# A decayed-attention and two-MLP kernel: blocks of up to 512 tokens, decays by scans, and a shorter first plan

## The chip, the cores and the metric

The kernel runs on one core of a Trainium2 chip. The metric is the device time of one execution in microseconds, as the median of several runs. A profile of one execution stands beside it, with the work of TensorE (PE), VectorE (DVE), ScalarE (ACT), GpSimd (POOL) and the DMA queue that SyncE (SP) issues.

## What is computed

Linear attention with a decay per key channel, then two MLPs, all in float32:

```python
# q, k, v, alpha: (4, 8, 768, 48); alpha in 0.8 to 1.0
for t in range(S):
    state = alpha[:, :, t, :, None] * state + np.einsum('bhd,bhe->bhde', k[:, :, t], v[:, :, t])
    y[:, :, t] = np.einsum('bhd,bhde->bhe', q[:, :, t], state)
x = y.transpose(0, 2, 1, 3).reshape(3072, 384)
h = x @ w_in                                   # 384 x 2048
x = (np.maximum(h, 0) + a * np.minimum(h, 0)) @ w_out
h = x @ w2_in
x = np.where(h >= 1, h, np.where(h <= -1, 0, (h + 1) ** 2 / 4)) @ w2_out
```

## The kernel before

**Units.** The sequence is cut into chunks of 128 tokens; a unit is one chunk of one batch with its eight heads, 24 units in all, six to a batch. Two heads lie in one tile, one on partitions 0 to 47 and one on 64 to 111, so four pairs. For a unit the running product of alpha over the chunk (prod) and its inverse (inv) are formed; q is multiplied by prod and k by inv; the scores are masked and multiplied by v; and a state of 48x48 per head is carried from chunk to chunk.

**Stages of a unit.** "product" and "product_end": seven doubling passes over prod (L218, after a copy L212), 112x256 each, on DVE (unit 2 on POOL). "inverse": the last column kept (p_last, L512), a reciprocal of every fourth column (L515), three passes that fill the columns between (L518), k times inv (L522), all DVE; POOL multiplies q by prod (L343). "scores": PE transposes k (L658) and forms the scores (L664), ACT copies k to token-major order (k_tok, L405), DVE masks (L528). "mix": PE forms the state sums (L674) and the outputs (L684 with the state, L688 with v), ACT copies the outputs (L411), DVE updates the state (L551, L555). "turn": PE transposes the outputs (L702), ACT rounds them into x_hi (L418), DVE subtracts for x_lo (L561). A batch's first unit has no L684; its last one has no L674, but has its key transposes.

**The MLPs.** A block is 384 tokens, three units. There are eight blocks in each layer, and a step is one tile of 128 hidden channels of a block, 16 steps to a block. Every float32 product is made of three float32r products, high part times low, high times high, low times high (L723 to L725). In a step PE does the hidden product of the step two ahead (nine matmuls of 384 columns into one of two h_ps banks) and then the output product of this step (nine more, into y_ps). Between them ACT takes a relu (L433), DVE combines (L568 in the first layer, L576 and L579 in the second), ACT rounds into g_hi (L439), and POOL subtracts into g_lo (L350). g32, g_hi and g_lo have four slots each. x_hi and x_lo have two, so a block's units are made while the block before is multiplied.

**The order.** Each engine works in the order of its program; semaphores tie the engines. In step f of a block every engine first does the unit stages that BLOCK_PLAN gives to the step, then its part of the activation of step f + 2:

```python
BLOCK_STAGES = {0: "product", 1: "product_end", 2: "inverse", 3: "scores", 4: "mix", 5: "turn"}
BLOCK_PLAN = [[(BLOCK_STAGES[f - 4 * j], j) for j in range(UPB) if f - 4 * j in BLOCK_STAGES] for f in range(FT)]
```

So unit j of the next block starts at step 4j, and its stages take six steps in a row. The three units of block 0 are made ahead of all products by FIRST_PLAN, with idle matmuls of PE between its stages (FILL, WARM).

**Weights.** Each weight tile (768 columns, input and output part) is loaded raw into w_raw (RAW = 3 slots), rounded into w_hi by ACT (L400), and its low parts are formed by POOL (L335, input part) and DVE (L503, output part). In block 0 one tile is split in each step; the second layer's tiles are split in the first layer's last block. The blocks but the first and last of a layer are loops of two block bodies. Outputs go to y_all and from there to memory after their block.

Of the kernel before, what the change touches and what calls it, by code (L numbers as in the profile page):

```python
# [10 lines left out]
P = 128  # L33
# [8 lines left out]
TOK = 384  # L42
UPB = TOK // CHUNK
BLOCKS = BATCH * SEQ // TOK
# [3 lines left out]
G_RING = 4  # L48
RAW = 3
AHEAD = 2  # L50
LEVELS = CHUNK.bit_length() - 1
SECOND = BLOCKS * FT

BLOCK_STAGES = {0: "product", 1: "product_end", 2: "inverse", 3: "scores", 4: "mix", 5: "turn"}
BLOCK_PLAN = [[(BLOCK_STAGES[f - 4 * j], j) for j in range(UPB) if f - 4 * j in BLOCK_STAGES] for f in range(FT)]

FIRST_PLAN = [("product", 0), ("product_end", 0), ("inverse", 0), ("product", 2), ("product_end", 2), ("product", 1),  # L60
              ("scores", 0), ("product_end", 1), ("inverse", 1), ("mix", 0), ("inverse", 2), ("scores", 1), ("turn", 0),
              ("mix", 1), ("scores", 2), ("turn", 1), ("mix", 2), ("turn", 2)]
BY_POOL = 2
SPARE = 2


WARM = 27
FILL = {("scores", 0): 3, ("mix", 0): 10, ("turn", 0): 6, ("turn", 1): 0, ("mix", 2): 2, ("turn", 2): 5}


def build_program(nc, qka, v, w, alpha, out):
    with ExitStack() as ctx:
# [7 lines left out]

        w_hi = sb("w_hi", [P, FT, WCOLS], F32R)
        w_lo = sb("w_lo", [P, FT, WCOLS], F32R)
        w_raw = sb("w_raw", [P, RAW, WCOLS])

        x_hi = sb("x_hi", [P, 2, KT, TOK], F32R)
        x_lo = sb("x_lo", [P, 2, KT, TOK], F32R)

        y_all = sb("y_all", [P, BLOCKS, KT, TOK])
        g32 = sb("g32", [P, G_RING, TOK])
# [14 lines left out]
        ident = sb("ident", [P, P])  # L104

        h_ps = [ctx.enter_context(nc.psum_tensor(f"h_ps{i}", [P, 512], F32)) for i in range(2)]
# [6 lines left out]
        unit_loaded = [sem(f"unit_loaded{i}") for i in range(3)]  # L113
        raw_loaded = [sem(f"raw_loaded{i}") for i in range(RAW)]
        slopes_loaded = sem("slopes_loaded")
        alpha_loaded = sem("alpha_loaded")
        slopes_set = sem("slopes_set")
        stored = sem("stored")
        pads_set = [sem(f"pads_set{i}") for i in range(3)]
        state_cleared = sem("state_cleared")  # L120
        ident_set = sem("ident_set")
        causal_set = sem("causal_set")
        w_hi_done = sem("w_hi_done")
        w_lo_in_done = sem("w_lo_in_done")
        w_lo_out_done = sem("w_lo_out_done")
        product_done = sem("product_done")
        first_done = sem("first_done")
        pool_product_done = sem("pool_product_done")
        pool_first_done = sem("pool_first_done")
        last_kept = sem("last_kept")  # L130
        inv_done = sem("inv_done")
# [13 lines left out]
        x_lo_done = sem("x_lo_done")  # L145
        h_done = sem("h_done")
# [8 lines left out]


        spare = y_all[:, BLOCKS - 2:].rearrange("p n m t -> p (n m t)")

        def qka_of(u):
            if u == SPARE:  # L160
                return spare[:, 0:3 * PAIRS * CHUNK].rearrange("p (x h t) -> p x h t", x=3, h=PAIRS)
            return qka_sb[:, u % 2]

        def v_of(u):
            return spare[:, 3 * PAIRS * CHUNK:3 * PAIRS * CHUNK + D_MODEL] if u == SPARE else v_sb[:, u % 2]

        def prod_of(u):

            if u != BY_POOL:
                return prod  # L170
            return y_all[:, BLOCKS - 3].rearrange("p m t -> p (m t)")[:, 0:PAIRS * CHUNK].rearrange(
                "p (h t) -> p h t", h=PAIRS)
# [9 lines left out]
        def out_bank(u):  # L182

            return y_ps[2] if u in (1, 2) else t_ps

        def product_of(u, levels):

            if u == BY_POOL:
                return pool_product_done, levels
            return product_done, LEVELS * (u - (u > BY_POOL)) + levels  # L190

        def product_stages(eng, turn, u, levels):

            done, first = (pool_product_done, pool_first_done) if u == BY_POOL else (product_done, first_done)
            out = prod_of(u)[0:ROWS]
            if levels[0] == 0:
                if u == 0:
                    eng.wait_ge(alpha_loaded, 32)
                else:
                    eng.wait_ge(loaded_of(u), at(turn, 48 * UPB, loads_of(u)))  # L200
                if u != BY_POOL:

                    ge(eng, q_scaled, turn, UPT, u)
                    ge(eng, k_scaled, turn, UPT, u)
                    ge(eng, last_kept, turn, UPT, u)
            for level in levels:
                half = 1 << level
                x, y = (t.rearrange("p h t -> p (h t)").rearrange("p (n two s) -> p n two s", two=2, s=half)
                        for t in (out if level else qka_of(u)[0:ROWS, 2], out))
                count = product_of(u, level)[1]  # L210
                if level == 0:
                    eng.tensor_copy(y[:, :, 0], x[:, :, 0]).then_inc(first, 1)  # L212
                else:
                    eng.wait_ge(done, at(turn, LEVELS * UPT, count))
                if level == 1:
                    eng.wait_ge(first, at(turn, UPT, count // LEVELS + 1))
# [589 lines left out]
```

## Time and profile before

| | us |
|---|---|
| median of 3 runs | 1038.96 |
| lowest, highest | 1036.35, 1043.89 |
| span of the profiled execution | 1046.5 |
| PE busy in it | 980.5 |
| DVE busy | 525.3 |
| POOL busy | 361.9 |
| ACT busy | 318.0 |

The span goes from the first to the last instruction of the profiled execution, which is an execution of its own and not one of the three. In rows of instructions the first number is the start in us from the span's start, the second the duration; a bracket gives the idle time of the engine before it and what ended it. PE rows overlap, since matmuls are pipelined: the time from start to start is what one costs. PE's float32 matmuls appear as two records each, those of float32r as one.

### The profile page before, as it was taken

The page shows a single profiled execution, that of the slowest core. Times are in us where ns is not written, and L with a number is a line of the kernel's source. Part 1 is how long each engine was busy: PE and PEld are TensorE (multiplying, and loading weights), DVE is VectorE, ACT ScalarE, POOL GpSimd, SP SyncE. Part 2 cuts the span into 40 slices and gives each one's busy share as a digit, 9 for nine tenths or more (in the row PEclk, how much of TensorE's full clock was granted, in tenths as well). Part 3 has the DMA queues.
Part 4 walks back from the last instruction along what each step waited for, and adds up shares of the span by engine and source line. Part 5 has one row for each costly group of instructions (what it writes and reads, how often), then busy time and mean ns, then how long its engine had stood idle before and what let it go on. Part 6 is the DMA issues. An engine that isn't in the chain of part 4 may idle for free.

```text
span 1046.5 us, 17070 instructions
## 1 busy us (share of the span) xinstructions
PE 980.5 (94%) x5970; PEld 961.8 (92%) x5970; DVE 525.3 (50%) x908; ACT 318.0 (30%) x673; POOL 361.9 (35%) x354
## 2 busy tenths in 40 slices
PE   7977799999999999989998999999999999999998
PEld 7877799898889898889897999999999999999998
DVE  8577666556457466367377244333333333333332
ACT  1332232222222222222232355333333333333232
POOL 4233332222232232223123287434343434333333
PEclk9888899998899898899899999999999999999999
DMA  5413211201111201302102032000000000000000
GB/s 136 106 61 91 61 31 31 53 9 32 41 22 34 56 2 31 58 4 54 37 1 76 1 107 90 2 23 1 24 1 23 0 23 0 23 0 23 0 24 23
DMA packets 14923, 37.02 MB, mean 35 GB/s; under 512 B 2224, under 2 KB 8368, under 8 KB 14864
## 3 DMA queue, kind: packets, MB, share of 16 engines
q1 hardware_dynamic: 14864, 36.19, 14.3%
q8 instruction: 42, 0.69, 0.3%
q14 instruction: 17, 0.14, 0.0%
HBM read 31.47 MB, written 4.72 MB: 35 GB/s over the span
## 4 chain that ended last, share of the span: by engine, by line
PE 76%; DVE 16%; issue 5%; DMA 1%; ACT 1%; POOL 1%; DVEq 0%; SPq 0%; POOLq 0%
PE h_ps L723 11%; PE h_ps L725 11%; PE h_ps L724 11%; PE y_ps L723 10%; PE y_ps L724 10%; PE y_ps L725 10%; DVE prod L218 4%; DVE inv L518 3%; PE a_ps L688 3%; PE a_ps L664 3%; DVE qka_sb L522 2%; DVE inv L515 2%; PE a_ps L684 2%; PE t_ps L658 1%; PE t_ps L674 1%
## 5 line engine op out<-in xcount | busy, mean ns | idle before, releaser
L350 POOL TENSOR_TENSOR g_lo<-g,g_hi 128x384 fp32r<-128x384 f32 x256 | 261.5, 1021 | 652.6 <-ACT g_hi L439 550.6
L433 ACT ACTIVATE g<-h_ps 128x384 f32<-128x384 f32 x256 | 126.0, 492 | 499.9 <-PE h_ps L725 499.9
L723 PE MATMUL h_ps<-x_lo,w_hi 128*128 128x384 f32 x768 | 269.6, 351 | 2.6 <-issue 2.6
L724 PE MATMUL h_ps<-x_hi,w_hi 128*128 128x384 f32 x768 | 262.9, 342 | 0.0
L725 PE MATMUL h_ps<-x_hi,w_lo 128*128 128x384 f32 x768 | 262.9, 342 | 0.0
L723 PE MATMUL y_ps<-g_lo,w_hi 128*128 128x384 f32 x768 | 259.2, 337 | 1.1 <-POOL g_lo L350 1.1
L724 PE MATMUL y_ps<-g_hi,w_hi 128*128 128x384 f32 x768 | 258.3, 336 | 0.0
L725 PE MATMUL y_ps<-g_hi,w_lo 128*128 128x384 f32 x768 | 257.7, 336 | 0.0
L576 DVE SCALAR_TENSOR_TENSOR g<-g 128x384 f32<-128x384 f32 x128 | 71.4, 558 | 244.8 <-ACT g L433 244.8
L723 PEld LDWEIGHTS h_ps<-x_lo,w_hi 128*128 128x128 f32 x768 | 148.4, 193 | 7.2 <-issue 5.8
L724 PEld LDWEIGHTS h_ps<-x_hi,w_hi 128*128 128x128 f32 x768 | 148.9, 194 | 0.0
L725 PEld LDWEIGHTS h_ps<-x_hi,w_lo 128*128 128x128 f32 x768 | 148.8, 194 | 0.0
L723 PEld LDWEIGHTS y_ps<-g_lo,w_hi 128*128 128x128 f32 x768 | 146.4, 191 | 1.9 <-POOL g_lo L350 0.9
L724 PEld LDWEIGHTS y_ps<-g_hi,w_hi 128*128 128x128 f32 x768 | 146.0, 190 | 0.0
L725 PEld LDWEIGHTS y_ps<-g_hi,w_lo 128*128 128x128 f32 x768 | 145.5, 189 | 0.0
L568 DVE SCALAR_TENSOR_TENSOR g<-g,slopes,h_ps 128x384 f32<-128x384 f32 x128 | 78.2, 611 | 126.0 <-ACT g L433 125.5
L439 ACT ACTIVATE g_hi<-g 128x384 fp32r<-128x384 f32 x256 | 132.8, 519 | 4.7 <-DVE g L568 3.9
L218 DVE TENSOR_TENSOR prod<-prod 112x256 f32<-112x256 f32 x138 | 85.7, 621 | 4.0
L579 DVE TENSOR_TENSOR g<-h_ps,g 128x384 f32<-128x384 f32 x128 | 71.3, 557 | 4.4
L658 PE MATMUL t_ps<-ident,qka_sb 112*128 112x112 f32 x88 | 16.0, 314 | 51.5 <-DVE qka_sb L522 51.5
L658 PEld LDWEIGHTS t_ps<-ident,qka_sb 112*128 112x128 f32 x88 | 10.4, 163 | 58.3 <-DVE qka_sb L522 53.1
L688 PE MATMUL a_ps<-v_sb,att 128*128 128x48 f32 x352 | 48.7, 266 | 0.7 <-DVE att L528 0.7
(83 smaller groups left out, 708.1 us busy)
## 6 DMA issues: line engine op xcount, KB each, us to landing
qka_sb<-qka SPq DMA_DIRECT2D x44, 288.0 KB, 4.7
w_raw<-w SPq DMA_DIRECT2D x32, 384.0 KB, 3.0
y<-y_all SPq DMA_DIRECT2D x24, 192.0 KB, 1.9
v_sb<-v SPq DMA_DIRECT2D x23, 192.0 KB, 4.8
y_all<-qka SPq DMA_DIRECT2D x2, 288.0 KB, 8.7
qka_sb<-qka SPq DMA_DIRECT2D x2, 192.0 KB, 3.5
qka_sb<-qka SPq DMA_DIRECT2D x2, 96.0 KB, 2.5
y_all<-v SPq DMA_DIRECT2D x1, 192.0 KB, 9.3
```

What stands on the lines that cost most here:

```text
L218: eng.tensor_tensor(y[:, :, 1], x[:, :, 1], left, ALU.mult).then_inc(done, 1)
L350: nc.gpsimd.tensor_tensor(g_lo[:, r], g32[:, r], g_hi[:, r].bitcast(F32), ALU.subtract).then_inc(g_lo_done, 1)
L433: nc.scalar.activation(g32[:, s % G_RING], h_ps[s % 2][:, 0:TOK], ACT.Relu, scale=-1.0 if s < SECOND else 0.5, bias=0.0 if s < SECOND else ...
L439: nc.scalar.activation(g_hi[:, s % G_RING], g32[:, s % G_RING], ACT.Copy).then_inc(g_hi_done, 1)
L568: nc.vector.scalar_tensor_tensor(out=g32[:, r], in0=g32[:, r], scalar=slopes[:, f:f + 1], in1=h_ps[s % 2][:, 0:TOK], op0=ALU.mult, op1=ALU ...
L576: nc.vector.scalar_tensor_tensor(out=g32[:, r], in0=g32[:, r], scalar=1.0, in1=g32[:, r], op0=ALU.min, op1=ALU.mult).then_inc(half_done, 1)
L579: nc.vector.tensor_tensor(g32[:, r], h, g32[:, r], ALU.max).then_inc(g_done, 1)
L658: last = nc.tensor.transpose(turn_bank(u)[:, h * P:h * P + ROWS], qka[0:ROWS, 1, h], ident[0:ROWS, 0:ROWS])
L688: last = nc.tensor.matmul(scores_bank(u, 0)[:, c], att[:, e, h], v_of(u)[:, c], start=fresh, stop=fresh or e == 1)
L723: nc.tensor.matmul(out_, wh, lo, start=start, stop=False)
L724: nc.tensor.matmul(out_, wh, hi, start=False, stop=False)
L725: last = nc.tensor.matmul(out_, wl, hi, start=False, stop=stop)
```

## The change

- Block sizes in units are (2, 3, 3, 4, 4, 4, 4) in the first layer and six of 4 in the second: 13 blocks and 208 steps instead of 16 and 256. A matmul of the products has 128 x size columns, 512 at most.
- Each unit's stages are planned back from its turn: decay 5 steps ahead, scores 3, mix 1. The last unit of a block turns at step 13 of the block before, the others 4 steps apart. Within a step the order is turn, scores, mix, decay.
- prod and inv come from scans: per unit four forward and four backward over 128 columns and a reciprocal of the last column of each pair. p_last is copied by POOL. No unit's product runs on POOL.
- The state sums go to the second scores bank instead of the turn bank. A batch's last unit has neither key transposes nor k_tok.
- FIRST_PLAN has two units; WARM and FILL are smaller. ACT splits weight tiles in between, ahead of copies of the plan; POOL makes both low parts of the first four tiles.
- g32 has two slots, g_hi and g_lo three. Raw weights of the first layer lie in eleven slots of y_all that is not yet written, those of the second layer in four slots where qka was.
- Loops are unrolled. The output array is (3, 128, 3072), with 512-byte pieces on the chip's side for each unit.
- SP loads unit u (from 2 on) when the outputs of unit u - 2 are done, instead of after its x_lo.

```diff
-TOK = 384
-G_RING = 4
-RAW = 3
+FIRST = (2, 3, 3, 4, 4, 4, 4)
+SECOND = (4, 4, 4, 4, 4, 4)
+SIZES = FIRST + SECOND
+TOK = CHUNK * max(SIZES)
+G32_RING, G_RING = 2, 3
+RAW_FIRST, RAW_SECOND = 11, 4
+EARLY = 4
-BLOCK_STAGES = {0: "product", 1: "product_end", 2: "inverse", 3: "scores", 4: "mix", 5: "turn"}
+for _n in range(1, N1):
+    for _j in range(SIZES[_n]):
+        _u, _turn = STARTS[_n] + _j, FT * (_n - 1) + 13 - 4 * (SIZES[_n] - 1 - _j)
+        for _stage, _lag in (("decay", 5), ("scores", 3), ("mix", 1), ("turn", 0)):
+            PLAN.setdefault(_turn - _lag, []).append((_stage, _u))
+ORDER = ("turn", "scores", "mix", "decay")
+FIRST_PLAN = [("decay", 0), ("decay", 1), ("scores", 0), ("scores", 1), ("mix", 0), ("turn", 0), ("mix", 1), ("turn", 1)]
+WARM = 20
+FILL = {("scores", 0): 3, ("scores", 1): 1, ("mix", 0): 4, ("mix", 1): 2, ("turn", 1): 3}
...
+            def decay(u):
+                al = qka_of(u)[0:ROWS, 2]
...
+                for h in range(PAIRS):
+                    nc.vector.tensor_tensor_scan(prod[0:ROWS, h], al[:, h], zeros[0:ROWS], 1.0,
+                                                 ALU.mult, ALU.add).then_inc(prod_done, 1)
+                dve.wait_ge(prod_done, PAIRS * (u + 1))
+                ge(dve, k_scaled, u)
+                nc.vector.reciprocal(inv[0:ROWS, :, CHUNK - 1], prod[0:ROWS, :, CHUNK - 1]).then_inc(inv_begun, 1)
+                dve.wait_ge(inv_begun, u + 1)
+                for h in range(PAIRS):
+                    nc.vector.tensor_tensor_scan(inv[0:ROWS, h, CHUNK - 2::-1], al[:, h, CHUNK - 1:0:-1],
+                                                 zeros[0:ROWS, 0:CHUNK - 1], inv[0:ROWS, h, CHUNK - 1:CHUNK],
+                                                 ALU.mult, ALU.add).then_inc(inv_done, 1)
...
                 nc.vector.tensor_tensor(k, k, inv[0:ROWS], ALU.mult).then_inc(k_scaled, 1)
...
+            splits = {("decay", 0): [0], ("decay", 1): [1, 2, 3]}
...
+                for i in splits.get(task, []):
+                    split_in(i)
+                    split_out(i)
...
+            splits = {("decay", 1): [0, 1], ("scores", 0): [2], ("scores", 1): [3], ("turn", 0): [4], ("turn", 1): [5]}
...
+            load_unit(0)
+            load_unit(1)
             sp.dma_start(slopes[:], alpha).then_inc(slopes_loaded, 16)
+            for i in range(6):
+                load_weights(i)
+            load_unit(2)
```

Of the two `splits`, the first is POOL's, after scale_q of the unit, and the second ACT's, after its own part of the stage.

## Rows read from the trace of the kernel before

**Rows 1.** The page: engines' busy time, and the granted clock in 40 slices.
```profile
PE 980.5 (94%) x5970; PEld 961.8 (92%) x5970; DVE 525.3 (50%) x908; ACT 318.0 (30%) x673; POOL 361.9 (35%) x354
...
PEclk9888899998899898899899999999999999999999
```

**Rows 2.** The view by stretches: start, first layer, second layer, tail.
```profile
core 0: us, PE busy (x) PEld busy (x) DVE busy (x) ACT busy (x) POOL busy (x), PEclk, DMA share, GB/s
...
42.90:646.10 603.20, 548.49 (x3423) 532.18 (x3422) 346.83 (x585) 177.78 (x367) 194.62 (x180) 0.93 0.20 46
646.10:1043.40 397.30, 396.70 (x2287) 396.06 (x2286) 146.72 (x264) 131.76 (x293) 151.98 (x151) 1.00 0.03 11
1043.40:1046.50 3.10, 0.00 (x0) 0.00 (x0) 0.04 (x1) 0.49 (x1) 0.00 (x0) 0.85 0.53 190
```

**Rows 3.** The waits of PE: total us, times, longest us.
```profile
PE t_ps L658 <- DVE qka_sb L522: 51.5, 21, 6.3
...
PE h_ps L723 <- issue: 2.6, 2, 1.5
```

**Rows 4.** Timeline of PE, one unit's stages at full clock.
```profile
170.37 0.60 PE L658 MATMUL t_ps<-ident,qka_sb 112*128 112x112 f32 x4 [1.22 <-DVE qka_sb L522]
170.90 1.16 PE L664 MATMUL a_ps<-qka_sb 48*128 48x128 f32 x16
172.00 0.44 PE L723 MATMUL h_ps<-x_lo,w_hi 128*128 128x384 f32 x1
...
175.23 0.93 PE L674 MATMUL t_ps<-v_sb,k_tok 128*112 128x96 f32 x8
176.00 0.39 PE L684 MATMUL a_ps<-state,qka_sb 112*128 112x96 f32 x2
...
178.62 0.42 PE L723 MATMUL h_ps<-x_lo,w_hi 128*128 128x384 f32 x1
...
181.83 0.49 PE L702 MATMUL t_ps<-ident,o_tok 128*128 128x128 f32 x3
182.08 0.42 PE L723 MATMUL h_ps<-x_lo,w_hi 128*128 128x384 f32 x1
```

**Rows 5.** Timeline of PE, the same stage behind a longer wait.
```profile
270.34 0.68 PE L658 MATMUL t_ps<-ident,qka_sb 112*128 112x112 f32 x4 [2.38 <-DVE qka_sb L522]
270.95 2.08 PE L664 MATMUL a_ps<-qka_sb 48*128 48x128 f32 x16
272.96 0.69 PE L723 MATMUL h_ps<-x_lo,w_hi 128*128 128x384 f32 x1
```

**Rows 6.** Groups by line and shape: busy us, mean ns, idle before.
```profile
L350 POOL TENSOR_TENSOR g_lo<-g,g_hi 128x384 fp32r<-128x384 f32 x256 | 261.5, 1021 | 652.6 <-ACT g_hi L439 550.6 <-issue 91.0 <-DVE g L568 10.9
...
L439 ACT ACTIVATE g_hi<-g 128x384 fp32r<-128x384 f32 x256 | 132.8, 519 | 4.7 <-DVE g L568 3.9 <-DVE g L579 0.8
...
L218 DVE TENSOR_TENSOR prod<-prod 112x256 f32<-112x256 f32 x138 | 85.7, 621 | 4.0
...
L568 DVE SCALAR_TENSOR_TENSOR g<-g,slopes,h_ps 128x384 f32<-128x384 f32 x128 | 78.2, 611 | 126.0 <-ACT g L433 125.5
...
L335 POOL TENSOR_TENSOR w_lo<-w_raw,w_hi 128x384 fp32r<-128x384 f32 x32 | 39.3, 1229 | 10.1 <-ACT w_hi L400 10.0
...
L518 DVE TENSOR_TENSOR inv<-inv,qka_sb 112x128 f32<-112x128 f32 x69 | 38.5, 557 | 2.4
...
L503 DVE TENSOR_TENSOR w_lo<-w_raw,w_hi 128x384 fp32r<-128x384 f32 x32 | 33.5, 1049 | 9.3 <-ACT w_hi L400 9.1
...
L522 DVE TENSOR_TENSOR qka_sb<-qka_sb,inv 112x512 f32<-112x512 f32 x23 | 22.3, 971 | 0.8
...
L515 DVE RECIPROCAL inv<-prod 112x128 f32<-112x128 f32 x23 | 21.8, 946 | 0.0
...
L218 DVE TENSOR_TENSOR prod<-qka_sb 112x256 f32<-112x256 f32 x23 | 10.4, 452 | 0.0
```

**Rows 7.** Timeline of DVE in the start: unit 1's decay begins, the last x_lo.
```profile
11.72 0.30 DVE L212 COPY prod<-qka_sb 112x256 f32<-112x256 f32 x1 [0.77 <-DMA v_sb<-v]
...
42.22 0.56 DVE L561 TENSOR_TENSOR x_lo<-y_ps,x_hi 128x384 fp32r<-128x384 f32 x1 [0.58 <-ACT x_hi L418]
```

More of the change, by code:

```diff
@@ L180, in turn_bank @@
             return y_ps[2] if u == 1 else t_ps
[L182 to L216, printed above, removed]
-                left = x[:, :, 0, half - 1:half].to_broadcast(x[:, :, 1].shape)
-                eng.tensor_tensor(y[:, :, 1], x[:, :, 1], left, ALU.mult).then_inc(done, 1)
@@ L359, in attention @@
-            def attention(turn, plan, first_unit):
-                for stage, j in plan:
-                    u = first_unit + j
-                    if stage == "product" and u == BY_POOL:
-                        product_stages(pool, turn, u, range(0, LEVELS))
-                    if stage == "inverse":
-                        scale_q(turn, u)
-            pool.wait_ge(pads_set[SPARE], 2)
-            attention(None, FIRST_PLAN, 0)
-            for i in range(RAW):
-                split_w(i)
@@ L373, in body @@
+            splits = {("decay", 0): [0], ("decay", 1): [1, 2, 3]}
+            for task in FIRST_PLAN:
+                if task[0] == "decay":
+                    scale_q(task[1])
+                for i in splits.get(task, []):
+                    split_in(i)
+                    split_out(i)
+            for n in range(BLOCKS):
                 for f in range(FT):
                     s = FT * n + f
-                    if n == 0 and f == 0:
-                        hidden_lo(turn, 0)
-                    if n == 0 and f + RAW < FT:
-                        split_w(f + RAW)
@@ L390, in _ @@
-            run(pool, body)
+                    if s == 0:
+                        hidden_lo(0)
+                    for stage, u in plan_of(s):
+                        if stage == "decay":
+                            scale_q(u)
+                    if s + 1 < STEPS:
+                        hidden_lo(s + 1)
+                    if n == 0 and f + EARLY < FT:
+                        split_in(f + EARLY)
+                    if N1 - 1 <= n < BLOCKS - 1 and 5 <= f < 5 + KT:
+                        input_lo(n + 1, f - 5)
@@ L452, in attention @@
[L452 to L464 removed]
+                    act.wait_ge(hidden_used, FT * (n + 1))
@@ L465, in _ @@
+            for stage, u in FIRST_PLAN:
+                if stage == "scores":
+                    copy_k(u)
+                if stage == "mix":
+                    copy_outputs(u)
+                if stage == "turn":
+                    turn_hi(u)
+                for i in splits.get((stage, u), []):
                     split_w(i)
             for s in range(AHEAD):
-                relu_of(None, s)
-            def body(turn, n):
+                relu_of(s)
+            for n in range(BLOCKS):
@@ L492, in _ @@
-            run(act, body)
-            copy_y(None, 2 * BLOCKS - 1, 0)
-            copy_y(None, 2 * BLOCKS - 1, 2)
+                        copy_y(n - 1, 0)
+                        copy_y(n - 1, 2)
+                    for stage, u in plan_of(s):
+                        if stage == "scores":
+                            copy_k(u)
+                        if stage == "mix":
+                            copy_outputs(u)
+                        if stage == "turn":
+                            turn_hi(u)
@@ L628, in body @@
+            for n in range(BLOCKS):
                 for f in range(FT):
@@ L642, in _ @@
-            run(dve, body)
-            copy_y(None, 2 * BLOCKS - 1, 1)
+                        copy_y(n - 1, 1)
+                    for stage, u in plan_of(s):
+                        if stage == "turn":
+                            turn_lo(u)
+                        if stage == "scores":
+                            mask(u)
+                        if stage == "mix":
+                            update_state(u)
+                        if stage == "decay":
+                            decay(u)
@@ L804 @@
     y = r.results[0]["y"]
[L805 removed]
+    return np.ascontiguousarray(y.reshape(D_MODEL, BATCH * SEQ).T)
```

664 lines of the change are left out of this document (321 added, 343 removed).

## The prediction

> **What bounds the kernel now.** I read the page first: PE (TensorE) is busy 94% of the span, and its granted clock dips from 1.0 to 0.8 or 0.9 in many slices of the first half and in none of the second [rows 1]. So TensorE sets the time, and the question is which of its microseconds are work. The view by stretches splits the span at three places of the trace: the first hidden product (42.9 us), the first matmul after the first layer's last output product (646.1 us) and the last matmul (1043.4 us) [rows 2]. The reader is to see that the two layers have the same matmuls (128 steps of 18) and that one takes 603.2 us, the other 397.3.
>
> The second layer gives the price of pure work: 397.3 us for 2,286 matmuls (2,304 less the 18 of the two steps issued ahead) is 173.8 ns for 384 columns, while the clock stays at 1.0, 2.4 GHz [rows 2]. 384 columns at 2.4 GHz are 160 ns, so 13.8 ns come on top of each matmul. The first layer's stretch holds 2,322 such matmuls, 403.6 us. The other 199.6 us are attention and loss.
>
> The attention work of one unit (128 tokens of one batch, all heads) is read off a unit at full clock, from start to start [rows 4]: key transposes 0.53 us, scores 1.10, state sums 0.77, outputs 2.62 (176.00 to 178.62), output transposes 0.25. Each return to the products costs 0.09 more, three times. That is 5.5 us. For a unit that opens a batch (no product with the state) it is 0.9 less, for one that closes it 0.8 less. The 21 units 3 to 23: 21 x 5.5 - 3 x 0.9 - 4 x 0.8 = 109.6 us.
>
> So 90 us of the first layer are lost. The waits of PE name 51.5 us of it: 21 waits, one per unit, of the key transposes for the scaled keys that DVE writes at L522, 6.3 us at most [rows 3]. Most of the rest is clock: behind a wait of 1.2 us the scores took 1.16 us, behind one of 2.4 us 2.08 us, and the first hidden matmul 0.69 instead of 0.44 [rows 4, 5]. TensorE had stood still before, and the records run at the lower level, 1.2 GHz. In the second layer, with no wait, nothing of that appears.
>
> Why is DVE late? A unit's decay work runs over three steps: seven products at L218 (the first 452 ns, the others 621), the reciprocal 946, three of L518 at 557, L522 971 [rows 6], with two short copies some 8.5 us in an engine that works in order. Between them it also stands behind the activations of the steps, which wait for hidden products that TensorE has yet to make. The scores come one step (3.13 us) after the last part.
>
> **The change, part by part.**
>
> *Decay by scans.* Seven doubling passes, the p_last copy and three inverse passes per unit leave DVE; 4 + 4 scans of 112x128, a reciprocal of 4 columns and the same L522 come. The trace has no scan. From below it is bounded by half of the first product (256 columns, 452 ns), 0.23 us; from above by the slowest row per column, the reciprocal of 128 columns, 0.95 [rows 6]. I take 0.45, between, and on the side of L518 (128 columns, 0.56 mean), because a scan divides nothing. Decay is then 8 x 0.45 + 0.16 (an estimate for the reciprocal of 4 columns, 946 less what 124 columns cost at 6 to 7 ns) + 0.97 = 4.7 us (2.9 to 8.7) in one piece. The Trainium skill, "DVE: opcode table, instruction layouts, handler registers and perf-mode slots", section "Datapath and trigger behaviour", says that this scan runs at half throughput. The trace of before has none to compare; by the page, 128 columns would take about what 256 take in a product, an estimate of 0.45.
>
> *Stages spaced apart.* Decay stands two steps ahead of the scores, and the scores two ahead of the mix. With four steps between units the decay of unit u+1 falls into the step of mix(u). Take T as this step's start on PE: outputs end at T+3.4, DVE's state update (four short ops, 1.5) at T+4.9, decay at T+9.6. PE reaches the scores two steps later: the mix 3.4 + two steps of products + the 0.3 of the turn. For 512-token blocks (step 4.1, below) that is T+11.9; for 384 (3.13) T+10.0; for 256 (2.2) T+8.1. So the wait is gone in the wide blocks, just gone at 384, and 1.5 us remain at the two units prepared that way in block 0. The activation queued on DVE behind the decay is needed a step later still: in a 384 block g is done at about T+10.2, g_lo 1.5 later (519 + 1,021 ns [rows 6]) at T+11.8, and the output product that needs it starts at T+13.2 (10.0 + 1.6 of scores + 1.6). Thin, no term. If this cover goes, every microsecond of decay more is a microsecond per unit. I leave 5 us of loss for block 0 and a cold start of the products. Gain 90 - 5 = 85.
>
> *Blocks of 512 with a ramp.* 13 blocks instead of 16: 208 steps, 3,744 matmuls instead of 4,608, the same columns. Whether the 13.8 ns is fixed per matmul or grows with the columns no row shows. Fixed (my choice: columns at 2.4 GHz should stream, something is paid at each change of weights): 512 takes 227 ns, the gain is 864 x 13.8 ns = 11.9 us. In proportion: 232 ns, gain nothing. Cost of the other engines at 512: ACT's copy 0.52 us to about 0.65 and the relu alike, DVE's combine 0.61 to 0.78, GpSimd's g_lo 1.02 to 1.36 [rows 6]; ACT has two of them in a step of 4.1, the others one. At 256, block 0 also splits weights: DVE 0.45 + 1.05 and GpSimd 0.7 + 1.23 in a 2.2 us step [rows 6], both near full, but TensorE has 16 us of attention in that block as cover. The Trainium skill, "TensorE: Matmul & The Clock Gate", section "Wait — 56ns, not 53.3ns?", has N/2.4 + 2.5 ns for a stream of matmuls: 162.5 at 384, where this trace has 173.8, so for this fp32r stream with a weight load each the measurement decides. By the page the 864 matmuls would be worth 2.2 us.
>
> *One unit moves from the start into the blocks, batch-closing units skip the key transposes.* 22 units instead of 21: +5.5. Closing units lose 4 x 0.53. Together +3.4.
>
> *The start.* Now unit 1's decay begins at 11.72, after a DMA had held it 0.77 us, and the third unit's x_lo at 42.22 releases the products at 42.92 [rows 7]. With two units: k of unit 0 scaled near 9, that of unit 1 near 14. But new queues form: ACT has splits 0 and 1 ahead of copy_k(0), and GpSimd has both halves of split 0 (2 x 1.23) ahead of scale_q(1), all behind the first weight's DMA, which is issued behind ten unit transfers and should land at 11 to 12. So scale_q(1) ends near 16, scores of unit 1 near 18.5 at the low clock, mix 0 at 22, o_tok and turn 24, mix 1 at 28, turn and x_lo of unit 1 near 31. First products at 31 (26 to 37) instead of 42.9: gain 11.9.
>
> *Weights staged in y space, RAW 3 to 11 and 4; unrolled; no third pad or POOL product.* The weights were in time already: PE waits for none of them [rows 3]. Nothing, hidden behind products. The loops leave no wait row on PE beyond a few "issue" microseconds [rows 3]; nothing, up to 3 us gain.
>
> *Tail.* The last copy and DMA are a third larger: 3.1 us [rows 2] to about 3.7, +0.6.
>
> Sum: 1046.5 - 85 - 11.9 + 3.4 - 11.9 + 0.6 = 941.7 us of span. The profiled span lies 7.5 us over the median of the runs (1038.96). The losses by waits and clock, which may differ from run to run, are nearly gone after, so I carry over only a little of that: **940 us**.
>
> **Rivals.**
> *A. The start stays long or block 0 binds.* For it: the new order on ACT and GpSimd above, and DVE near full in block 0. Against: two units instead of three. The start keeps its 42.9 and block 0 loses 5 more: 940 + 11.9 + 5 = 957 us.
> *B. Scans at the reciprocal's 0.95 us.* Decay 8.7: waits of 1.7 us at the 12 units prepared in 512 steps, 3.6 at 7 in 384, 5.5 at 3 in 256, 62 us, and some 15 of lower clock as now: 1017 us. Against: no division in a scan.
> *C. The 13.8 ns do not exist at 512 columns.* 2,880 wide matmuls x 13.8 = 40 us less: 900 us. The page's gap formula points this way, but the row at 384 speaks against it. The opposite, growth in proportion, is 952 us and inside the range.
> *D. Slower than before: the shorter rings.* g32 has two slots instead of four, so relu of step s+2 waits for g_lo of step s. The chain from h(s) to g_lo(s) is 0.65 + 0.78 + 0.65 + 1.36 = 3.4 us, and 8.2 us (two steps) are there. It decides from 8.2 on; the 105 us that lead back to 1046 need 0.5 us more in each of 208 steps, a chain of 9.2 us; at 9.3 it is 1,056 us. The decay in front of the activation reaches it once per unit, not per step.
>
> **Numbers.** Forecast case 0.70, A 0.18, B 0.05, C 0.04, D 0.02, the change not doing what it says (waits as now) 0.01. The range 922 to 966 holds the forecast with starts 26 to 37, a matmul price up to the proportional one and a decay up to 6 us, and reaches over A. Measurement of this kernel tells about 1% from no change. Faster by over 1%: 0.96 (all but D and part of B), within 1% 0.02, slower 0.02.
>
> **What would show it.** Key transposes without wait of over 1 us outside block 0; scores at 1.1 us throughout and the clock at 1.0 from about 35 us on; 512-column matmuls 227 ns apart; scan rows of 0.3 to 0.6 us; first hidden product at 26 to 37 us; the second layer 1,728 matmuls in about 391 us. Wrong if PE waits for g_lo or for a weight, if the scans take near 1 us, or if the clock dips with no wait in front of it.

## The result

The changed kernel takes 979.26 us (median of 4 runs, 975.71 to 981.99); the kernel before, run beside it, 1041.17. The ratio is 0.9414, 95% interval 0.9373 to 0.9455. The forecast was 940 us (922 to 966): the direction was right, about three fifths of the gain came, and the time lies outside the range. The span of the profiled execution is 980.3 us; the working of the prediction ended at 941.7.

| us | predicted | measured |
|---|---|---|
| start, to the first hidden product | 31 | 36.4 |
| products, 3,744 matmuls | 789 | 788.2 |
| attention of 22 units at full clock | 113 | 113 (taken as such) |
| waits and low clock between the products | 5 | 38.8 |
| tail | 3.7 | 3.9 |
| span | 941.7 | 980.3 |

The 788.2 us of products have two parts. The second layer's stretch below is 388.6 us, for 1,710 matmuls of 512 columns. The first layer's is priced from start to start of one matmul in the trace: 120 ns for 256 columns, 173.3 for 384, 226.7 for 512. It holds 288, 576 and 1,170 of them (18 of the last are the second layer's first two steps, issued ahead), 399.6 us. The 38.8 us are what is left of the first layer's 551.4 us (587.8 less 36.4) after these 399.6 and the 113 of attention.

The page of the changed kernel, engines' busy time and granted clock in 40 slices; it answers to [rows 1].

```profile
PE 946.6 (97%) x5050; PEld 815.9 (83%) x5050; DVE 448.1 (46%) x732; ACT 302.8 (31%) x561; POOL 354.8 (36%) x322
...
PEclk8777999999999999999999999999999999999999
```

The dips of the first half are gone, but for the first four slices. The view by stretches (start; block 0; the rest of the first layer; the second layer) shows the same, and answers to [rows 2].

```profile
core 0: us, PE busy (x) PEld busy (x) DVE busy (x) ACT busy (x) POOL busy (x), PEclk, DMA share, GB/s
0.00:36.40 36.40, 29.68 (x169) 28.31 (x169) 15.86 (x35) 8.83 (x13) 14.43 (x24) 0.72 0.69 196
36.40:113.20 76.80, 64.59 (x472) 61.66 (x472) 47.52 (x81) 24.57 (x55) 29.92 (x34) 0.84 0.27 62
113.20:587.80 474.60, 464.25 (x2704) 405.28 (x2703) 248.59 (x420) 147.57 (x277) 165.92 (x152) 1.00 0.20 42
587.80:976.40 388.60, 388.07 (x1711) 320.67 (x1709) 136.07 (x198) 121.26 (x218) 144.57 (x113) 1.00 0.04 11
```

Block 0 takes 76.8 us. Its products are 37.7 (288 matmuls of 256 columns, and 18 of 384 that belong to the first two steps of block 1) and its three units 16.5, so 22.6 of the 38.8 us are lost there: PE stands still for 12.2 of them, and the rest goes with a mean clock of 0.84. Blocks 1 to 5 have a stretch of their own:

```profile
113.20:522.50 409.30, 398.95 (x2415) 351.22 (x2414) 221.44 (x388) 116.53 (x225) 123.20 (x119) 1.00 0.19 37
```

With 296.6 us of products and 19 units at 5.5, the other 16.2 us are lost there, at full clock. PE stands still for 10.4 of them, in small waits; for the other 5.8 no view names a cause, and they may be units that cost somewhat more than 5.5 us. Block 6, with no unit in it, loses nothing (65.3 us for 288 matmuls).

The waits of PE in the changed kernel, total us, times, longest; they answer to [rows 3].

```profile
PE t_ps L607 <- DVE x_lo L518: 12.7, 12, 3.0
PE y_ps L670 <- POOL g_lo L303: 8.8, 10, 1.7
PE y_ps L607 <- POOL qka_sb L294: 4.7, 1, 4.7
PE t_ps L607 <- DVE qka_sb L480: 1.9, 2, 1.4
```

The 51.5 us of waiting for scaled keys have become 1.9. In their place stand two waits that were absent or small before (1.1 us for g_lo, none for x_lo): the key transposes for x_lo of the unit before (they write the bank t_ps from which DVE still has to form it), and the output products for g_lo. The third line of the four is one wait in the start.

The timelines of DVE and of POOL in the changed kernel, in the first step of block 5, which holds a mix and a decay.

```profile
440.51 0.74 DVE L511 TENSOR_TENSOR state<-state,p_last 48x192 f32<-48x192 f32 x2
441.28 1.37 DVE L467 TENSOR_TENSOR_SCAN prod<-qka_sb,zeros 112x128 f32<-112x128 f32 x4
442.69 0.18 DVE L471 RECIPROCAL inv<-prod 112x4 f32<-112x4 f32 x1
442.90 3.90 DVE L474 TENSOR_TENSOR_SCAN inv<-qka_sb,inv,zeros 112x127 f32<-112x127 f32 x4
446.84 0.69 DVE L480 TENSOR_TENSOR qka_sb<-qka_sb,inv 112x512 f32<-112x512 f32 x1
447.56 0.75 DVE L524 SCALAR_TENSOR_TENSOR g<-g,slopes,h_ps 128x512 f32<-128x512 f32 x1
448.23 0.55 DVE L518 TENSOR_TENSOR x_lo<-t_ps,x_hi 128x384 fp32r<-128x384 f32 x1
```

```profile
442.73 1.29 POOL L294 TENSOR_TENSOR qka_sb<-qka_sb,prod 112x512 f32<-112x512 f32 x1 [6.02 <-DVE prod L467]
443.96 0.20 POOL L297 COPY p_last<-prod 112x4 f32<-112x4 f32 x1
444.10 1.30 POOL L303 TENSOR_TENSOR g_lo<-g,g_hi 128x512 fp32r<-128x512 f32 x1
```

Two things are to be seen. POOL stood 6.02 us in front of scale_q (L294) until the forward scans had run, and g_lo of the next step was queued behind it. And four forward scans take 1.37 us, four reverse ones 3.90: beside the reverse ones POOL is at work from their start at 442.90 to 445.40, 2.5 us. In the start, with POOL quiet, four reverse scans took 1.60:

```profile
10.54 1.60 DVE L474 TENSOR_TENSOR_SCAN inv<-qka_sb,inv,zeros 112x127 f32<-112x127 f32 x4
```

The activation (L524) and x_lo (L518) follow only after the decay.

### The profile page after: what moved, and what is told of

It is laid out like the page before. It is cut to its first block, busy times and chain, and to the rows that moved or that the text cites. A ratio compares the mean times of both kernels' runs of the same rounds, so it can differ in the third digit from the quotient of the medians.

```text
span 980.3 us, 13041 instructions
## 1 busy us (share of the span) xinstructions
PE 946.6 (97%) x5050; PEld 815.9 (83%) x5050; DVE 448.1 (46%) x732; ACT 302.8 (31%) x561; POOL 354.8 (36%) x322
## 4 chain that ended last, share of the span: by engine, by line
issue 43%; PE 32%; POOL 20%; DVE 3%; DMA 1%; SPq 0%; ACT 0%; POOLq 0%; DVEq 0%; ACTq 0%
POOL g_lo L303 16%; PE h_ps L670 4%; PE y_ps L670 4%; PE y_ps L672 4%; PE y_ps L671 4%; PE h_ps L672 4%; PE h_ps L671 4%; PE a_ps L640 2%; POOL x_lo L310 2%; POOL w_lo L283 2%; PE a_ps L616 1%; PE a_ps L636 1%; PE a_ps L628 1%; DVE prod L467 1%; DVE inv L474 1%
## 5 line engine op out<-in xcount | busy, mean ns | idle before, releaser
L303 POOL TENSOR_TENSOR g_lo<-g,g_hi 128x512 fp32r<-128x512 f32 (+2 forms) x208 | 251.7, 1210 | 507.5 <-ACT g_hi L391 503.9
L384 ACT ACTIVATE g<-h_ps 128x512 f32<-128x512 f32 (+2 forms) x208 | 117.6, 565 | 493.9 <-PE h_ps L672 475.4
L670 PE MATMUL y_ps<-g_lo,w_hi 128*128 128x512 f32 (+2 forms) x624 | 234.4, 376 | 8.9 <-POOL g_lo L303 8.8
L670 PE MATMUL h_ps<-x_lo,w_hi 128*128 128x512 f32 (+2 forms) x624 | 240.9, 386 | 0.1
L672 PE MATMUL h_ps<-x_hi,w_lo 128*128 128x512 f32 (+2 forms) x624 | 234.2, 375 | 0.0
L671 PE MATMUL h_ps<-x_hi,w_hi 128*128 128x512 f32 (+2 forms) x624 | 233.9, 375 | 0.0
L672 PE MATMUL y_ps<-g_hi,w_lo 128*128 128x512 f32 (+2 forms) x624 | 233.3, 374 | 0.0
L671 PE MATMUL y_ps<-g_hi,w_hi 128*128 128x512 f32 (+2 forms) x624 | 233.3, 374 | 0.0
L524 DVE SCALAR_TENSOR_TENSOR g<-g,slopes,h_ps 128x512 f32<-128x512 f32 (+2 forms) x112 | 74.8, 669 | 142.9 <-ACT g L384 142.3
L391 ACT ACTIVATE g_hi<-g 128x512 fp32r<-128x512 f32 (+2 forms) x208 | 123.2, 592 | 31.3 <-DVE g L524 29.0
L474 DVE TENSOR_TENSOR_SCAN inv<-qka_sb,inv,zeros 112x127 f32<-112x127 f32 x96 | 81.2, 903 | 0.9
L294 POOL TENSOR_TENSOR qka_sb<-qka_sb,prod 112x512 f32<-112x512 f32 x24 | 30.8, 1284 | 103.9 <-DVE prod L467 101.0
```

The lines of the kernel that those rows point to most:

```text
L294: nc.gpsimd.tensor_tensor(q, q, prod[0:ROWS], ALU.mult).then_inc(q_scaled, 1)
L303: nc.gpsimd.tensor_tensor(g_lo[:, s % G_RING, 0:w_], g32[:, s % G32_RING, 0:w_], g_hi[:, s % G_RING, 0:w_].bitcast(F32), ALU.subtract).the ...
L384: nc.scalar.activation(g32[:, s % G32_RING, 0:w_], h_ps[s % 2][:, 0:w_], ACT.Relu, scale=-1.0 if first else 0.5, bias=0.0 if first else 0. ...
L391: nc.scalar.activation(g_hi[:, s % G_RING, 0:w_], g32[:, s % G32_RING, 0:w_], ACT.Copy).then_inc(g_hi_done, 1)
L474: nc.vector.tensor_tensor_scan(inv[0:ROWS, h, CHUNK - 2::-1], al[:, h, CHUNK - 1:0:-1], zeros[0:ROWS, 0:CHUNK - 1], inv[0:ROWS, h, CHUNK - ...
L524: nc.vector.scalar_tensor_tensor(out=g32[:, r, 0:w_], in0=g32[:, r, 0:w_], scalar=slopes[:, f:f + 1], in1=h_ps[s % 2][:, 0:w_], op0=ALU.mu ...
```

## The experiments

The theory after this comparison: the place of the decay, in the step of the mix, costs the changed kernel its remaining gain, by two queues (g_lo behind scale_q on POOL; activation and x_lo behind the decay on DVE) and by POOL's work beside the scans. The rivals: the scans are long by themselves; the ring of two g32 slots; wide blocks' worth; the clock in the start. A ratio is to the kernel before, timed beside the run. Stretches and waits are those of one profiled execution of each kernel, and two executions of one kernel can lie some microseconds apart.

**The order on POOL.**

```diff
-                    for stage, u in plan_of(s):
-                        if stage == "decay":
-                            scale_q(u)
                     if s + 1 < STEPS:
                         hidden_lo(s + 1)
+                    for stage, u in plan_of(s):
+                        if stage == "decay":
+                            scale_q(u)
```

> The changed kernel with one order turned round on GpSimd: in a step with a decay, g_lo of the next step comes before scale_q, not behind it. Queue theory: scale_q waits up to 6 us for the forward scans, and g_lo stands behind it, so the 10 waits of the output products for g_lo (8.8 us) and the 10 waits of relu for g_lo (18.5 us on ACT) go; the key transposes' 12.7 us of waits for x_lo stay within 4 us, block 0 keeps its low clock in part; 979 falls to 966 to 974 us. Length theory (the decay on DVE is simply too long): the output products wait for g_lo as before because g itself is late, 977 to 981 us.

Measured: 972.79 us, 0.9314 (0.9275 to 0.9353). The waits for g_lo are nearly gone (ACT's relu, too, waits 0.9 us for it instead of 18.5), those for x_lo have grown by 4.2 us, slightly more than expected.

```profile
PE t_ps L607 <- DVE x_lo L518: 16.9, 12, 4.7
...
PE y_ps L670 <- POOL g_lo L303: 0.8, 2, 0.5
```

The queue was real, but what lay behind it came forward: blocks 1 to 5 fell from 409.3 to 407.1 us and block 0 from 76.8 to 72.9; 2.7 us more come from an earlier start (33.7 us) with the same code there (below).

**POOL quiet beside the reverse scans.** On top of the last edit:

```diff
                 pool.wait_ge(prod_done, PAIRS * (u + 1))
+                if u >= 2:
+                    pool.wait_ge(inv_done, PAIRS * (u + 1))
```

> As a1_glo_first, and scale_q (from unit 2 on) also waits for the unit's reverse scans, so GpSimd is quiet while they run. Contention theory: four reverse scans take 1.6 us as in the start, not 3.2 to 4.0; decay ends some 2 us earlier, the waits of the key transposes (12.7 us) fall under 4 us, and 950 to 962 us result. Theory that the reverse scans are long by themselves in the blocks: they stay at 3.2 to 4.0, q comes later and the key transposes wait more, 975 to 990 us.

Measured: 961.42 us, 0.9201 (0.9164 to 0.9238). The reverse scans' group in the changed kernel and in this one, mean ns of one, and a reverse group with one POOL instruction beside it:

```profile
L474 DVE TENSOR_TENSOR_SCAN inv<-qka_sb,inv,zeros 112x127 f32<-112x127 f32 x96 | 81.2, 903 | 0.9
```

```profile
L476 DVE TENSOR_TENSOR_SCAN inv<-qka_sb,inv,zeros 112x127 f32<-112x127 f32 x96 | 51.3, 594 | 0.9
```

```profile
423.81 2.60 DVE L476 TENSOR_TENSOR_SCAN inv<-qka_sb,inv,zeros 112x127 f32<-112x127 f32 x4
...
423.93 1.45 POOL L305 TENSOR_TENSOR g_lo<-g,g_hi 128x512 fp32r<-128x512 f32 x1 [6.32 <-ACT g_hi L393]
```

The contention theory holds, and with a size: four reverse scans take 1.60 us alone, 1.0 more with 1.45 us of POOL beside them, 2.3 more with 2.5 (above). They don't come down to 1.6 everywhere, since g_lo now runs where scale_q ran. The waits left are 7.2 us for x_lo, both in block 0, where under 4 had been expected, and 3.0 for q. Blocks 1 to 5: 399.3 us. The Trainium skill, "SBUF — State Buffer", section "SBUF: two separate sides", says that a VectorE instruction with two SBUF inputs and a GpSimd instruction that reads SBUF hold a port pair in turn, and that the other one "fully blocks". The rows agree in kind, not in full: in most groups of the changed kernel and of this one between six and nine tenths of POOL's time beside them are lost to the scans (1.0 of 1.45 us and 2.3 of 2.5 in the rows shown), not all of it. POOL's own durations are rough.

**The decay a step earlier, with the two edits above.**

```diff
-        for _stage, _lag in (("decay", 5), ("scores", 3), ("mix", 1), ("turn", 0)):
-            PLAN.setdefault(_turn - _lag, []).append((_stage, _u))
+        for _stage, _lag in (("decay", 6), ("scores", 3), ("mix", 1), ("turn", 0)):
+            PLAN.setdefault(max(_turn - _lag, 0), []).append((_stage, _u))
```

> As a2_quiet, and the decay stands six steps ahead of the turn, not five: a step without mix, so x_lo of the unit before no longer stands behind it on DVE. Place theory (x_lo behind decay and a late activation is what the key transposes wait for): their waits of 3.6 us in block 0 go to under 1, the low clock in block 0 with them, block 0 takes 58 to 63 us instead of 69.1 and the whole 946 to 954 against 961.4. Load theory (in block 0 DVE has too much in a step of 2.2 us, weight splits among it, wherever the decay stands): the waits only move, 958 to 965.

Measured: 949.5 us, 0.9118 (0.9074 to 0.9162), as the place theory has it. Block 0 and blocks 1 to 5:

```profile
30.30:90.80 60.50, 56.80 (x472) 54.94 (x473) 48.55 (x87) 24.61 (x55) 31.98 (x34) 0.97 0.41 102
90.80:488.00 397.20, 395.91 (x2416) 352.29 (x2415) 213.50 (x383) 114.86 (x225) 130.32 (x119) 1.00 0.19 39
```

**The place alone.** The changed kernel with nothing but that edit.

> The changed kernel with one number changed: the decay six steps ahead of the turn instead of five; GpSimd's order and the scans beside its work stay. Place theory: out of the step of the mix, scale_q waits less long for the scans and g_lo behind it is in time, x_lo is no longer behind the decay, so most of the gain of the three edits of a3_decay_early (979 to 949) comes from this one: 952 to 961. Length theory (the contention of scans and GpSimd must go too): 962 to 975.

Measured: 957.1 us, 0.9193 (0.9156 to 0.9229). One number is worth 22 us. The reverse scans are as long as before (920 ns against 903), the forward ones are longer, since g_lo now runs beside them (601 ns in the mean against 442), and it hardly matters:

```profile
L474 DVE TENSOR_TENSOR_SCAN inv<-qka_sb,inv,zeros 112x127 f32<-112x127 f32 x96 | 82.8, 920 | 0.9
...
L467 DVE TENSOR_TENSOR_SCAN prod<-qka_sb,zeros 112x128 f32<-112x128 f32 x96 | 52.1, 601 | 1.6 <-DMA qka_sb<-qka 1.4 <-POOL p_last L297 0.2
```

```profile
36.10:103.50 67.40, 61.61 (x472) 59.29 (x472) 51.40 (x86) 24.58 (x56) 30.13 (x35) 0.90 0.30 71
103.50:503.40 399.90, 397.57 (x2416) 353.63 (x2415) 234.53 (x383) 114.90 (x225) 123.53 (x119) 1.00 0.18 38
```

So contention costs most where the decay stands in a tight place, and the place is worth more than the other two edits: with them it is another 8 us. Blocks 1 to 5 are within 2.7 us of the last kernel's; block 0, with steps of 2.2 us, still wants the quiet scans.

**The ring.**

```diff
-G32_RING, G_RING = 2, 3
+G32_RING, G_RING = 4, 3
```

> The changed kernel with four g32 slots instead of two. Ring theory: the 18.5 us in which ACT's relu waits for g_lo come from the short ring and delay the activations; without them 965 to 974 us. Queue theory: g_lo itself is late behind scale_q on GpSimd, relu stands behind DVE's decay anyway, and nothing moves, 976 to 981.

Measured: 974.07 us, 0.9342 (0.9298 to 0.9387), between the two expectations, so the trace has to tell. ACT's waits for g_lo, in the changed kernel and here:

```profile
ACT g L384 <- POOL g_lo L303: 18.5, 10, 2.6
```

```profile
ACT g L384 <- POOL g_lo L303: 1.1, 1, 1.1
```

But blocks 1 to 5 take 409.3 us in both kernels, and the waits of PE are 12.7 and 8.8 us in both. The difference lies in the start (33.5 us against 36.4) and in block 0 (75.0 against 76.8), that is in the clock. Relu was released earlier, but the copy behind it on ACT then waited longer for DVE's activation (36.5 us instead of 29.0), which stands behind the decay.

**Blocks of 384 in the changed kernel.**

```diff
-FIRST = (2, 3, 3, 4, 4, 4, 4)
-SECOND = (4, 4, 4, 4, 4, 4)
+FIRST = (2, 3, 3, 3, 3, 3, 3, 4)
+SECOND = (3, 3, 3, 3, 3, 3, 3, 3)
```

> The changed kernel with blocks of 384 tokens all through except the first (256) and the last of the first layer (512): 16 blocks, 256 steps. Per-matmul theory: 864 more matmuls of the fixed 13.7 ns, layer 2 is 399 us instead of 389, 11 to 13 us in all, 990 to 993. Cover theory: besides, 12 units are prepared in steps of 3.1 instead of 4.1 us and lose 2.5 us each as in blocks 1 and 2, not 1: 12 to 18 us more, 1000 to 1010.

Measured: 991.92 us, 0.9520 (0.9474 to 0.9567). From the first hidden product to the last matmul it is 954.3 us against 940.0: 14.3 more, of which 864 matmuls at 13.4 ns are 11.6. But block 0, the same program in both, took 73.9 us here and 76.8 there, by its clock. Behind it the difference is 17.2 us, which leaves 5.6 for the shorter cover; PE's waits for g_lo have grown by 3.1 us, to 11.9. The per-matmul theory holds, and of the 12 to 18 us of the cover theory a third to a half at most is there.

**The kernel before, with the stages spaced only.** The scores stand two steps behind the inverse instead of one, and units are loaded when the outputs are done, a part that no run tests by itself.

```diff
-BLOCK_STAGES = {0: "product", 1: "product_end", 2: "inverse", 3: "scores", 4: "mix", 5: "turn"}
-BLOCK_PLAN = [[(BLOCK_STAGES[f - 4 * j], j) for j in range(UPB) if f - 4 * j in BLOCK_STAGES] for f in range(FT)]
+BLOCK_STAGES = {0: "product", 1: "product_end", 2: "inverse", 4: "scores", 5: "mix", 6: "turn"}
+OFFSETS = (0, 4, 7)
+BLOCK_PLAN = [[(BLOCK_STAGES[f - OFFSETS[j]], j) for j in range(UPB) if f - OFFSETS[j] in BLOCK_STAGES] for f in range(FT)]
...
-                    sp.wait_ge(x_lo_done, 1 if u == SPARE + 2 else done)
+                    sp.wait_ge(outputs_done, 1 if u == SPARE + 2 else done)
```

> The kernel before with nothing but the stages spaced: scores, mix and turn one step later, units starting at steps 0, 4 and 7 of a block, and the loads of units released by the outputs instead of x_lo. Spacing theory: the waits for scaled keys (51.5 us) and the low clock behind them are what the spacing removes; one step is 3.1 us and more than 18 of the 21 waits (2.5 us at most) vanish, the three of block 0 (6 us) halve; 1041 falls to 965 to 985 us. Scan theory (DVE's nine us of decay work is the cause wherever the scores stand): the waits move but stay, 1020 to 1045 us.

Measured: 974.86 us, 0.9328 (0.9291 to 0.9365), four microseconds under the whole change. The 51.5 us of [rows 3] read here:

```profile
PE t_ps L659 <- DVE qka_sb L523: 3.2, 3, 2.4
```

and from block 1 to the end of the first layer the clock stays at 1.00:

```profile
43.30:124.30 81.00, 75.84 (x466) 73.24 (x466) 57.67 (x91) 29.97 (x57) 36.44 (x33) 0.93 0.32 81
124.30:573.30 449.00, 445.45 (x2960) 437.29 (x2960) 275.57 (x495) 147.96 (x309) 159.88 (x148) 1.00 0.19 43
```

The doubling passes, all of DVE's 8.5 us a unit, are still there. What cost was that the scores stood too close behind them.

**The kernel before, with the scans only.** Unit 2's product also moves from POOL to DVE, and the order of the start with it.

```diff
...
-                left = x[:, :, 0, half - 1:half].to_broadcast(x[:, :, 1].shape)
-                eng.tensor_tensor(y[:, :, 1], x[:, :, 1], left, ALU.mult).then_inc(done, 1)
+            for h in levels:
+                eng.tensor_tensor_scan(out[:, h], qka_of(u)[0:ROWS, 2, h], zeros[0:ROWS], 1.0,
+                                       ALU.mult, ALU.add).then_inc(done, 1)
```

(and the reverse scans, as in the change, in its inverse stage.)

> The kernel before with nothing but the decays by scans (forward scans in its product stage, reverse scans in its inverse stage, unit 2 on DVE too). Scan theory: DVE's work for a unit falls from 8.5 to 4 to 6 us, the inverse stage from 4.3 to 2.5 to 4 us, so the waits of 1.4 us go and those of 2.5 shrink to under 1; with the clock 1041 falls to 975 to 1000 us. Spacing theory: the scores stand one step behind the inverse in the same order and the gain stays under 25 us, 1016 to 1040 us.

Measured: 1011.71 us, 0.9692 (0.9649 to 0.9736), between the two: 33 us. The start is 5.5 us shorter (37.4), and 35.9 us of waits for keys remain:

```profile
PE t_ps L657 <- DVE qka_sb L521: 35.9, 21, 3.9
```

**Both edits on the kernel before.**

> The kernel before with both edits, stages spaced and decays by scans, blocks of 384 throughout and the old start of three units. If the two remove the same waits, the sum of their gains (70 and 33 us) isn't had: with the waits gone by spacing, scans give only the faster start (b2_scans started its products at 37.4 instead of 42.9) and block 0's rest, 962 to 970 us against 974.9. If they are independent: 935 to 945.

Measured: 960.82 us, 0.9238 (0.9204 to 0.9272), near what was expected for two remedies of the same waits (962 to 970), and a little better. The start is 38.5 us against 43.3, block 0 is 74.1 against 81.0, and blocks 1 to 7 are 446.8 against 449.0. With blocks of 384, three units ahead and loops, this is 18 us faster than the changed kernel.

**The start.** The start of the changed kernel is the same program in a1, a2, a3, a7, c1 and r4, and the first hidden product came at 33.7, 33.5, 30.3, 36.1, 32.3 and 33.5 us. PE's timeline there, first in the changed kernel:

```profile
16.05 0.92 PE L607 MATMUL y_ps<-ident,qka_sb 112*128 112x112 f32 x4 [4.70 <-POOL qka_sb L294]
...
19.50 1.67 PE L628 MATMUL a_ps<-v_sb,k_tok 128*112 128x96 f32 x8
...
20.97 3.33 PE L640 MATMUL a_ps<-v_sb,att 128*128 128x48 f32 x15
```

A wait of 4.7 us, then every matmul at half pace, until 36.4 us. In a3_decay_early, the same program up to there, the pace came back at 21 us, and the 16 records of the last line (L642 there) took 1.91 us:

```profile
20.86 1.91 PE L642 MATMUL a_ps<-v_sb,att 128*128 128x48 f32 x16
```

The edit fills the wait:

```diff
-FILL = {("scores", 0): 3, ("scores", 1): 1, ("mix", 0): 4, ("mix", 1): 2, ("turn", 1): 3}
+FILL = {("scores", 0): 20, ("scores", 1): 1, ("mix", 0): 4, ("mix", 1): 2, ("turn", 1): 3}
```

First on top of the three edits:

> As a3_decay_early, with 20 instead of 3 idle matmuls behind the scores of unit 0, about as long as the 4.6 us that PE waits there for q of unit 1. Clock theory of the start: PE never stands still before the mix of unit 0, the matmuls run at 2.4 GHz throughout, the first hidden product comes at 26.5 to 28.5 us in place of 30.3 (33.5 in three of the other kernels, 36.4 in the changed one), and the total falls by 2 to 5 us with less spread. Otherwise (the drop comes from the narrow matmuls of the mix themselves): low clock in the mix as before and no gain.

Measured: 945.8 us, 0.9098 (0.9068 to 0.9128), the fastest kernel of the study, with runs from 945.67 to 946.52 where a3 had 947.43 to 951.59. The first hidden product comes at 28.1 us and the clock never falls:

```profile
17.91 0.93 PE L630 MATMUL a_ps<-v_sb,k_tok 128*112 128x96 f32 x8
18.68 1.91 PE L642 MATMUL a_ps<-v_sb,att 128*128 128x48 f32 x16
```

```profile
0.00:28.10 28.10, 24.28 (x202) 22.83 (x203) 16.53 (x35) 8.82 (x13) 14.64 (x24) 1.00 0.73 203
28.10:89.10 61.00, 55.50 (x471) 53.44 (x472) 49.81 (x86) 24.68 (x56) 31.35 (x34) 1.00 0.41 102
```

Then on the changed kernel alone:

> The changed kernel with 20 instead of 3 idle matmuls behind the scores of unit 0 and nothing else. Clock theory: the start alone cost the changed kernel 2 to 8 us by the lower clock, from execution to execution; with the gap filled the first hidden product comes at 28 to 29 us as in a5_start_filled instead of 36.4, block 0 keeps its waits of 3 us and its low clock, and 969 to 975 us result. If block 0's low clock also comes from the start: it goes with it, 958 to 965.

Measured: 971.12 us, 0.9305 (0.9247 to 0.9363). The first hidden product comes at 28.1, and block 0 takes 76.8 us as in the changed kernel: its low clock is made by its own waits.

**An attempt at the start that failed.** On top of the three edits, POOL splits tile 0 after scale_q of unit 1, ACT rounds tiles 0 and 1 after k of unit 0 is copied and tile 2 after k of unit 1, and there are more idle matmuls in each gap:

```diff
-FILL = {("scores", 0): 3, ("scores", 1): 1, ("mix", 0): 4, ("mix", 1): 2, ("turn", 1): 3}
+FILL = {("scores", 0): 8, ("scores", 1): 2, ("mix", 0): 8, ("mix", 1): 4, ("turn", 1): 5}
```

> As a3_decay_early, with the start reordered: GpSimd scales q of unit 1 before it splits weight tile 0, ACT copies k of unit 0 before it rounds tiles 0 and 1, and more idle matmuls fill PE's gaps. Queue theory of the start: the scores of unit 1 begin near 13 us instead of 16 and the matmuls of the start run at 2.4 GHz, so the first hidden product comes at 26 to 29 us instead of 33.5, and 5 to 7 us go from the total. DMA theory (weights and unit 1 arrive too late for more): under 2 us.

Measured: 951.98 us, 0.9135 (0.9093 to 0.9177), no faster than without; neither theory's time of the first hidden product was met, it came at 32.8 us. The wait went from q to k:

```profile
10.18 1.27 POOL L296 TENSOR_TENSOR qka_sb<-qka_sb,prod 112x512 f32<-112x512 f32 x1 [1.59 <-DVE prod L469]
...
10.35 3.20 DVE L476 TENSOR_TENSOR_SCAN inv<-qka_sb,inv,zeros 112x127 f32<-112x127 f32 x4
...
14.94 0.60 PE L609 MATMUL y_ps<-ident,qka_sb 112*128 112x112 f32 x4 [2.66 <-DVE qka_sb L482]
```

scale_q now ran beside the reverse scans, which took 3.20 us instead of 1.60, so the scores of unit 1 began 1.0 us earlier, not 3. And the idle matmuls behind mix 0 lasted 3.05 us where the next stage was ready after 0.7.

## Why the prediction was wrong

*What bounds the kernel.* Right. TensorE with 90 us of waits and their low clock was the place of the gain, and spacing alone gave 70 us (b1_spaced). The price of pure work held for layers and widths.

*Blocks of 512, fixed 13.8 ns.* Right: 512 columns are 226.7 to 227.3 ns, 13.4 to 13.9 over the columns, all products together came to 788.2 us where 789 were forecast, and the way back to 384 cost what 864 of them cost and 5.6 us more (c1_all_384). Rival C, that the cost vanishes at 512, fell. The Trainium skill's gap formula, N/2.4 + 2.5 ns, which the prediction quotes, would give 215.8 ns there, an estimate; it doesn't hold for this stream.

*Decay by scans, 4.7 us.* Mis-sized, and for another reason than the one weighed. Alone a scan takes 0.34 us forward and 0.40 reverse, less than the 0.45 taken, and the unit's decay 3.9 us in the start. (The reciprocal of 4 columns was put at 0.16 us by 6 to 7 ns a column, which no row of before shows; it took 0.18, and from 4 to 128 columns that is 6.2 ns a column.) The Trainium skill's half rate of this scan ("DVE: opcode table, instruction layouts, handler registers and perf-mode slots", section "Datapath and trigger behaviour") is neither shown nor refuted by that; the estimate of 0.45 from it and the 256-column product was too high. In the blocks the decay took 5.6 to 7.0 us, because scale_q and g_lo run beside the scans. The trace of before had this: L522 took 0.69 us with POOL idle in the start and 0.97 in the mean [rows 6]. The prediction put the 0.97 into the sum as a constant, and it is a price that depends on what the other engine does. The row of the start, in the trace of before:

```profile
10.26 0.69 DVE L522 TENSOR_TENSOR qka_sb<-qka_sb,inv 112x512 f32<-112x512 f32 x1
```

Rival B's 0.95 us came true for the reverse scans (903 ns mean) with a fraction of B's cost, since keys were not what came late.

*Stages spaced apart.* This is the step that failed. It priced the decay's end against the scores' need for keys, and the activation of step s + 2 against its output product, and called the second "thin, no term". Keys were in time indeed (1.9 us of waits), and behind block 0 no key transpose waited over 0.8 us for anything, as the prediction's signs have it. Not followed were two others in the same queues: on POOL, g_lo of step s + 1, which stands behind scale_q and so behind mix, state update and forward scans; on DVE, x_lo of the unit that turns one step later, which stands behind decay and activation while the next key transposes wait for its bank. They are the 8.8 and 12.7 us of the new waits, and the first of them is one of the prediction's own signs of being wrong. In a 384 block (the step from 163.3 us) the decay ended 10.8 us after the step's start, not 9.6, and x_lo 11.9, where PE would have come at 10.5 without its own wait for g_lo.

*Loss of 5 us.* It was 38.8, and that is nearly the whole miss; the start adds 5.4. Of the 38.8, 22.6 are block 0, where waits of up to 3 us come once a unit and the clock falls behind them: the same mechanism that the first part had read from before, and which the working didn't apply to its own 1.5 us waits. Moving the decay out of the mix's step took 9.4 us from block 0 and 9.4 from blocks 1 to 5 (a7_place_alone); with the two other edits it is 16.3 and 12.1 (a3_decay_early).

*The start, 31 us.* The queues came as worked out (scale_q of unit 1 ended at 15.9, "near 16"; scores at 18.9, "near 18.5"). The clock did not: mix 1 and the turns ran at half pace as well, to 36.4 us. The range of 26 to 37 held it, and a6_fill_only shows its size, 8 us.

*Rival A* (long start, block 0 binds, 957 us) was right in kind and not in size: the start took 36.4 us where it had 42.9, and block 0 lost 22.6 where it had 5 us more than the forecast case. *Rival D* (the ring) fell by r4_ring. How much of the difference the named parts explain is shown by a5_start_filled: with POOL's order, its work beside the scans, the place and the start mended, the kernel runs in 945.8 us, so these four are worth 33 of the 39 us between forecast and measurement. Left open is the rest, with block 0 of that kernel: 61.0 us against 54.2 of products and attention.

## What to carry to other kernels

When a stage moves, walk every queue that it stands in, one instruction past it, and ask who waits for that one; the instruction whose input was late before is the one thing that will be in time. Distance was worth more than speed here: one more step between producer and consumer gave 70 us with the slow decay and 22 with the fast one, where the fast decay alone gave 33. Price an operation by what its neighbour does meanwhile, and fill a gap of the matmul engine with idle matmuls up to its length and not beyond: 20 of them in a 4.7 us gap gave 8 us (a6_fill_only), too many behind mix 0 held up the next stage by over 2 (a4_start).

## What the runs showed of the hardware

- Four reverse scans of 112x127 take 1.60 us alone, 2.60 beside one GpSimd instruction of 1.45 us (a2_quiet), 3.90 beside 2.5 us of them (the changed kernel); GpSimd's own instruction also lengthens, 1.29 us to 1.75 beside L482 on DVE in a2_quiet.
- Once the clock had fallen behind the 4.7 us wait, it stayed at the lower level with PE at work on the scores, the mix and the turns: at half pace from 16 us to 36 in the changed kernel, to 21 in a3_decay_early, with the same program. The first hidden products lie 6 us apart (36.4 and 30.3).
- float32r matmuls with a weight load each cost their columns at 2.4 GHz plus 13.3 to 13.9 ns, at 256, 384 and 512 columns alike (120.0, 173.3 and 226.7 ns from start to start in the changed kernel).
